# Folding the gate weights in full columns, with the spatial weights in one transfer

## The chip, the cores and the metric

The kernel runs on one core of a Trainium2 chip. The metric is the device time of one execution in microseconds (us), as the median of several runs; lower is better. The engines are TensorE (PE in the profile, its weight loads PEld), VectorE (DVE), ScalarE (ACT), GpSimd (POOL) and SyncE (SP). All arithmetic is float32.

## The reference

Three stages run one behind the other. The first is a recurrence over 768 time steps for 4 batches of 8 heads of width 40, the second a gated layer with a spatial mix, the third a routed layer with eight experts. Cut to what matters:

```python
def _attn_ref(r, k, v, w, a, b):                 # y: [4, 8, 768, 40]
    for t in range(S):
        y[:, :, t] = einsum('bhd,bhde->bhe', rt, state)
        Sa = einsum('bhde,bhe->bhd', state, at)
        state = state * wt - outer(Sa, bt) + outer(vt, kt)

def _moe_ref(x, w_in, w_spatial, b_spatial, w_out):
    h = maximum(x @ w_in, 0.0); u, v = halves of h            # 512 each
    v_n = (v - mean(v)) / sqrt(var(v) + 1e-6)
    v_s = einsum('ts,bsd->btd', w_spatial, v_n) + b_spatial[None, :, None]
    return (u * v_s) @ w_out                                  # [4, 768, 320]

def _moe2_ref(x, w_gate, w_local, w1, w2):
    logits = x @ w_gate; local_gate = sigmoid(x @ w_local)    # 8 and 1 columns
    e = argmax(logits) where fresh, otherwise the expert of the token before
    out = softmax(logits)[e] * (maximum(x @ w1[e], 0) @ w2[e])
```

## The kernel before

**The recurrence** (lines 948 to 1458) is cut into 24 chunks of 32 time steps. TensorE runs a loop of one step for each chunk (line 1175): small products with names like `unknowns`, `level`, `growth`, `scores_r`, `outputs`. In the profile a step takes 13.2 us. The other engines run the same chunks written out. SP loads each chunk's inputs (kb, a, vt, own, w, r and, last in a step, rg), each in a buffer of its own that is freed in the step. ScalarE copies banks of PSUM to SBUF (`drain`, line 1237), among them the state turned for the outputs, which also waits until rg has landed (line 1263). At one fixed place of each chunk it issues one part of the weights of the next stage (lines 1268 to 1272): `load` at line 124 has the spatial weights in six parts, `w_in` in four; `load_out` at line 139 the ten parts of the output and gate weights. VectorE masks the scores (line 1419) and scales the outputs (line 1455, it counts `y_d`).

**The end of the recurrence** is written out for TensorE in lines 1192 to 1215. Here the last chunk's products are mixed with the first products of the gated stage. `values` (line 230) multiplies two tiles of 128 tokens with the second half of `w_in` as a pair (`pair`, line 216): the full rows of the first tile, then whatever `between` holds, the full rows of the second tile, then the 64 remaining rows of both at line 227, side by side. Each tile of x waits for its own semaphore `x_tile`. The banks G and E of the first pair must have been read by ScalarE (`relu_v`, line 324) before the second pair writes them. The last tile of x is known only after the last outputs: `y_d`, then SP's `store` (line 935), then `load_tile` (line 938), and behind it on SP the bias and the first experts' weights. `gates` (line 247) multiplies the first half of `w_in`, with x streaming.

**The fold** (lines 163 to 190) computes w_out times the gate weights, a matrix of 512 rows by 9 columns (eight logits and one local gate), so that the output products of line 317 give the logits with the rows. w_out's transpose is in `woutT`, the nine columns in `wgl`, in three chunks of the 320 features (128, 128 and 64 rows). Twelve products load `wgl` as the stationary side and stream 128 columns of `woutT`, in four strips of 32 partitions of bank A. ScalarE copies the strips to SBUF (line 180), TensorE turns them (line 184), and ScalarE copies the result behind w_out (line 188). GpSimd adds the last weights for the mix behind this copy (line 269), since they take the place of `woutT`. The mix (`mix`, line 291) is the fourteen products of line 305.

The order in every engine's queue is the order in which the program is written. No scheduler moves anything.

Of the kernel before, what the change touches and what calls it, by code (L numbers as in the profile page):

```python
# [12 lines left out]
ACT = mybir.ActivationFunctionType  # L13
AX = mybir.AxisListType

P = 128
BATCH, HEADS, SEQ, HD = 4, 8, 768, 40
DM = HEADS * HD
# [5 lines left out]
EXPERTS = 8  # L24
# [51 lines left out]
class Gated:  # L76
# [4 lines left out]
    def __init__(self, nc, ctx, room, side, banks, x_rows, w_in, w_spatial, b_spatial, w_out, w_gate, w_local):  # L81
# [28 lines left out]
        self.transfers = TILES + 1 + NK  # L110
        self.strips, self.strips_clear = side.xTt[:, 0, 0, :], sem("strips_clear")
# [12 lines left out]
    def load(self, eng, part):  # L124
        w_in, w_spatial, b_spatial, w_out, w_gate, w_local = self.sources
        pairs = [(self.wspT[:, t, :], w_spatial[t * P:(t + 1) * P, :]) for t in range(TILES)]
# [36 lines left out]
    def fold(self, pe, woutT, wgl, bank, done):  # L163

        pe.wait_ge(self.out_loaded, 16 * self.OUT_PARTS)
        for k, (lo, rows) in enumerate(KCH):
            for d in range(ND):
                mm = pe.matmul(bank[self.strip(d), 0:P], wgl[0:rows, k, :], woutT[0:rows, k, d * P:(d + 1) * P],
                               start=(k == 0), stop=(k == NK - 1), skip_group_check=True)
        mm.then_inc(done, 1)  # L170

    def strip(self, d):

        return slice(d * 32, d * 32 + EXPERTS + 1)

    def copy_strips(self, act, bank, folded, done):
        act.wait_ge(folded, 1)
        act.wait_ge(self.strips_clear, 1)
        for d in range(ND):
            act.activation(self.strips[self.strip(d), :], bank[self.strip(d), 0:P], ACT.Copy).then_inc(done, 1)  # L180

    def turn_fold(self, pe, bank, ident, copied, done):
        pe.wait_ge(copied, ND)
        pe.transpose(bank[:, P:2 * P], self.strips, ident[:, :]).then_inc(done, 1)

    def copy_fold(self, act, bank, turned, done):
        act.wait_ge(turned, 1)
        act.activation(self.wout[:, :, DM:ROW],
                       bank[:, P:2 * P].rearrange("p (d n) -> p d n", n=32)[:, :, 0:EXPERTS + 1],
                       ACT.Copy).then_inc(done, 1)  # L190
# [39 lines left out]
    def values(self, pe, b, i, between=None):  # L230

        if b == 0:
            pe.wait_ge(self.x_tile[i], 16 * (NK + 1))
        if b >= 1 and i == 0:
            pe.wait_ge(self.x_full, 16 * (NK + 1) * b)

        def second():
            if between:
                between()
            if b == 0:  # L240
                pe.wait_ge(self.x_tile[i + 1], 16 * (NK + 1))

        self.pair(pe, self.v_at(b, i), D_HALF,
                  lambda g, k, rows: self.xT[rows, k, (i + g) * P:(i + g + 1) * P],
                  lambda g, k, rows: self.win[rows, k, D_HALF:], second)
# [1571 lines left out]
```

## Time and profile before

| | us |
|---|---|
| median of 3 runs | 933.83 |
| lowest and highest | 932.93, 934.34 |
| the profiled execution | 933.83 |
| its span, first to last instruction | 932.1 |
| TensorE busy in the span | 915.0 |
| recurrence, to the first values product | 347.5 |
| from there to the first gates product | 14.4 |
| from there to the first product of the mix | 19.1 |
| the rest: mix, batches 1 to 3, experts | 551.2 |

The span is what one execution took between its first and last instruction; the time of a run holds 1.7 us more. In the rows of the timeline the first number is the start in us from the span's start, the second how long the group lasted, then engine, line, operation and operands, and in brackets how long the engine was idle before it and what ended that. A float32 product shows as two passes, so x24 are twelve products.

### The profile page before, as it was taken

To read this page: it belongs to the slowest core of one execution; us is meant where nothing else is said; L and a number is where in the kernel's file an instruction comes from. 1 tells how busy PE (TensorE), PEld (TensorE's weight loads), DVE (VectorE), ACT (ScalarE), POOL (GpSimd) and SP (SyncE) were. 2 spreads that over 40 slices of the span, in tenths; PEclk is the share of its full clock that TensorE was granted. 3 is DMA by queue.
4 is the path that set the end of the run, shared out by engine and by line. 5 is a ranking of instruction groups with operands and counts; after the bars stand their busy time and mean duration, and the time that the engine had idled before them with its cause. 6 is when DMAs were issued, how large, how long until landed. Compare 5 with 4: busy or idle time off the path is not lost.

```text
span 932.1 us, 54066 instructions
## 1 busy us (share of the span) xinstructions
PE 915.0 (98%) x24654; PEld 710.4 (76%) x24655; DVE 477.5 (51%) x1026; ACT 251.5 (27%) x531; POOL 256.1 (27%) x232
## 2 busy tenths in 40 slices
PE   7999999999999999999999999999999999999997
PEld 6899999999999984545545545568888888888885
DVE  5478777877787643745455455463352222222230
ACT  0244444444444432102112112112212121212120
POOL 6454555455545551000020020020350111111011
PEclk8899999999999999999999999999999999999999
DMA  4235554554454322950110110329221110101000
GB/s 118 67 128 165 164 159 152 168 153 127 122 153 133 98 73 56 322 165 1 52 42 1 51 43 0 112 90 322 71 94 37 33 39 28 30 23 35 29 30 4
DMA packets 61477, 86.01 MB, mean 92 GB/s; under 512 B 22786, under 2 KB 41038, under 8 KB 61424
## 3 DMA queue, kind: packets, MB, share of 16 engines
q1 hardware_dynamic: 37232, 63.30, 22.2%
q10 hardware_dynamic: 21168, 13.32, 5.3%
q0 software_dynamic: 3024, 8.72, 2.6%
q8 instruction: 28, 0.46, 0.2%
q14 instruction: 25, 0.20, 0.1%
HBM read 72.47 MB, written 14.45 MB: 93 GB/s over the span
## 4 chain that ended last, share of the span: by engine, by line
PE 98%; issue 1%; ACT 0%; DVE 0%; POOL 0%; DVEq 0%; POOLq 0%; ACTq 0%
PE ps_D L1610 14%; PE ps_D L305 8%; PE ps_G L1592 6%; PE ps_E L1592 6%; PE ps_B L317 6%; PE ps_E L1096 5%; PE ps_A L305 4%; PE ps_B L223 3%; PE ps_G L1599 3%; PE ps_E L1094 3%; PE ps_D L1131 3%; PE ps_D L1068 3%; PE ps_G L223 3%; PE ps_D L1170 3%; PE ps_E L223 3%; PE ps_A L1073 2%
## 5 line engine op out<-in xcount | busy, mean ns | idle before, releaser
L1610 PE MATMUL ps_D<-room,hT 128*128 x496 | 138.8, 433 | 0.0
L1610 PEld LDWEIGHTS ps_D<-room,hT 128*128 128x128 f32 x496 | 91.9, 190 | 34.7
L1553 POOL DMA_INDIRECT out<-y,token x31 | 34.8, 1123 | 254.9 <-DVE y L1718 184.0
L661 POOL DMA_INDIRECT sorted_rows<-rows,slot x24 | 23.9, 995 | 237.7 <-DVE slot L653 231.6
L1718 DVE TENSOR_SCALAR y<-ps_D,x_in 128x320 f32<-128x320 f32 x31 | 17.0, 549 | 125.5 <-PE ps_D L1610 125.5
L1654 ACT ACTIVATE hT<-ps_G 128x512 f32<-128x512 f32 x31 | 18.5, 598 | 216.1 <-PE ps_E L1599 216.1
L1701 DVE COPY w_own<-room 128x1024 f32 x62 | 44.3, 720 | 63.0 <-PE ps_G L1592 34.4
L1350 DVE STREAM_TRANSPOSE room<-room 128x256 f32<-128x256 f32 x96 | 42.3, 441 | 48.1 <-ACT room L1237 48.1
L1592 PEld LDWEIGHTS ps_G<-xTt,w_own 128*128 128x128 f32 x496 | 60.0, 192 | 5.3 <-issue 1.0
L1592 PE MATMUL ps_G<-xTt,w_own 128*128 128x128 f32 x496 | 60.6, 275 | 0.6 <-ACT hT L1654 0.6
L1592 PE MATMUL ps_E<-xTt,w_own 128*128 128x128 f32 x496 | 60.5, 275 | 0.0
L1592 PEld LDWEIGHTS ps_E<-xTt,w_own 128*128 128x128 f32 x496 | 57.9, 192 | 0.0
L1019 POOL TENSOR_TENSOR room<-room 128x640 f32<-128x640 f32 x23 | 46.4, 2019 | 30.4 <-DVE room L1398 30.4
L317 PE MATMUL ps_B<-room 128*128 128x329 f32 x192 | 54.6, 441 | 0.0
L1237 ACT ACTIVATE room<-ps_E 128x256 f32<-128x256 f32 (+1 forms) x96 | 35.0, 365 | 66.9 <-PE ps_E L1096 36.6
L995 POOL TENSOR_TENSOR room<-room 128x1024 f32<-128x1024 f32 x24 | 52.2, 2176 | 1.9
L1030 POOL TENSOR_TENSOR room<-room 128x256 f32<-128x256 f32 x24 | 15.7, 656 | 125.7 <-DVE room L1442 125.7
L317 PEld LDWEIGHTS ps_B<-room 128*128 128x128 f32 x192 | 36.0, 190 | 18.4 <-issue 2.3
L1237 ACT ACTIVATE room<-room 128x512 f32<-128x512 f32 (+2 forms) x72 | 40.2, 558 | 34.5 <-PE ps_B L1148 31.2
L1096 PE MATMUL ps_E<-room 32*32 32x48 f32 (+1 forms) x3200 | 48.0, 205 | 1.5 <-issue 1.5
L1096 PEld LDWEIGHTS ps_E<-room 32*32 32x32 f32 x3200 | 40.6, 104 | 7.0 <-issue 6.0
L1237 ACT ACTIVATE room<-ps_D 128x1024 f32<-128x1024 f32 x24 | 24.6, 1026 | 48.6 <-PE ps_D L1068 48.6
(260 smaller groups left out, 1769.8 us busy)
## 6 DMA issues: line engine op xcount, KB each, us to landing
room<-in_moe_w SPq DMA_DIRECT2D x8, 1280.0 KB, 14.0
room<-in_moe_w SPq DMA_DIRECT2D x8, 1024.0 KB, 11.3
room<-in_vt SPq DMA_DIRECT2D x24, 320.0 KB, 3.8
room<-in_kb SPq DMA_DIRECT2D x46, 160.0 KB
x_in<-sorted_rows ACTq DMA_DIRECT2D x27, 161.0 KB, 2.2
room<-in_vo SPq DMA_DIRECT2D x24, 160.0 KB, 4.0
room<-in_rg SPq DMA_DIRECT2D x48, 80.0 KB
room<-in_r SPq DMA_DIRECT2D x48, 80.0 KB
```

Source lines behind the costliest of these rows:

```text
L223: pe.matmul(self.bank_of(n + g)[:, 0:width], left(g, k, slice(0, P)), right(g, k, slice(0, P)), start=(k == 0), stop=False, skip_group_che ...
L305: mm = pe.matmul(self.vs_bank[n % 3][:, 0:TH], left[:, s, c * P:(c + 1) * P], right[:, s, :], start=(s == 0), stop=(s == ST - 1))
L317: mm = pe.matmul(self.o_bank[n % 2][:, 0:ROW], self.g[:, d, i * P:(i + 1) * P], self.wout[:, d, :], start=(d == 0), stop=(d == ND - 1))
L995: pool.tensor_tensor(kb_end.rearrange("p m n k t -> p (m n) k t"), raw_kb[:, :, :, :], later[:, :, None, :].broadcast_to([P, GROUPS, 2, CH ...
L1019: pool.tensor_tensor(faded.rearrange("p m n e -> p (m n) e")[:, :, 0:HD], stateT.rearrange("p m n e -> p (m n) e"), whole[:, x % 4, :, Non ...
L1096: mm = pe.matmul(E[q, :, i, kept], pw[q, i, :], powers[q, l - 2:ROUNDS - 1:ROUNDS - l, i, kept], start=True, stop=True)
L1237: act.activation(out, in_, ACT.Copy).then_inc(done, 1)
L1350: dve.transpose(pw.rearrange("p i t -> p (i t)"), (powers[:, l - 1] if l else qi[:, 0]).rearrange("p i t -> p (i t)")).then_inc(flip_d[l], 1)
L1553: pool.indirect_dma_start(out=self.out[:, :], out_offset=bass.IndirectOffsetOnAxis(ap=side.token[:, u:u + 1], axis=0), in_=side.y[:, u % 2 ...
L1592: mm = pe.matmul(self.ps_h[half][:, f, :], side.w1_own[:, k, col:col + P], x[:, k, :], start=(f == 0 and k == 0), stop=False, skip_group_c ...
L1610: mm = pe.matmul(self.ps_y[:, u % 2], side.hT[:, u % 2, f, :], self.weights.w2[:, bass.ds(e, 1), f, :], start=(f == 0), stop=(f == self.NF ...
L1701: dve.tensor_copy(side.w1_own[:, :, cols], w1.w1[:, bass.ds(e, 1), :, cols].rearrange("p o k f -> p (o k) f")).then_inc(self.w1_in, 1)
```

## The change

Three things are edited. The six transfers of the spatial weights become one of 2304 KB, issued in the place of the first, so that the later parts of the weights are each issued five steps earlier. The fold loads `woutT` as the stationary side, 128 columns at a time, and streams the nine columns of `wgl`; its result stands on all 128 partitions as it is wanted, and the strips, their copies, the turning and the fill of the strips go. On TensorE the scores of the last chunk come in front of the second pair of values, the last outputs between its halves, and each pair of values waits for both of its tiles at its start.

```diff
-        self.transfers = TILES + 1 + NK
-        self.strips, self.strips_clear = side.xTt[:, 0, 0, :], sem("strips_clear")
+        self.transfers = 2 + NK
...
-        pairs = [(self.wspT[:, t, :], w_spatial[t * P:(t + 1) * P, :]) for t in range(TILES)]
+        pairs = [(self.wspT[:, :, :], w_spatial.rearrange("(t p) s -> p t s", p=P))]
...
-        for k, (lo, rows) in enumerate(KCH):
-            for d in range(ND):
-                mm = pe.matmul(bank[self.strip(d), 0:P], wgl[0:rows, k, :], woutT[0:rows, k, d * P:(d + 1) * P],
-                               start=(k == 0), stop=(k == NK - 1), skip_group_check=True)
+        for d in range(ND):
+            for k, (lo, rows) in enumerate(KCH):
+                mm = pe.matmul(bank[:, d, 0:EXPERTS + 1], woutT[0:rows, k, d * P:(d + 1) * P], wgl[0:rows, k, :],
+                               start=(k == 0), stop=(k == NK - 1))
...
-    def copy_strips(self, act, bank, folded, done):
+    def copy_fold(self, act, bank, folded, done):
         act.wait_ge(folded, 1)
...
-    def turn_fold(self, pe, bank, ident, copied, done):
...
+        act.activation(self.wout[:, :, DM:ROW], bank[:, :, 0:EXPERTS + 1], ACT.Copy).then_inc(done, 1)
...
-        if b == 0:
-            pe.wait_ge(self.x_tile[i], 16 * (NK + 1))
+        for t in (i, i + 1):
+            if b == 0:
+                pe.wait_ge(self.x_tile[t], 16 * (NK + 1))
...
-                pool.memset(gated.strips, 0.0).then_inc(gated.strips_clear, 1)
...
-                gated.fold(pe, woutT, wgl, A[:, 1], folded)
-                gated.values(pe, 0, 2, lambda: scores_r(now))
-                pe.wait_ge(kt_d, CHUNKS)
-                pe.wait_ge(rvu_d, now)
-                outputs(now)
-                pe.wait_ge(routing.consts, routing.CONSTANTS)
-                gated.turn_fold(pe, A[:, 1], side.ident, strips_d, fold_turned)
+                gated.fold(pe, woutT, wgl, A[:, 1].rearrange("p (d n) -> p d n", n=P), folded)
+                scores_r(now)
+
+                def final_outputs():
+                    pe.wait_ge(kt_d, CHUNKS)
+                    pe.wait_ge(rvu_d, now)
+                    outputs(now)
+
+                gated.values(pe, 0, 2, final_outputs)
...
-                gated.relu_v(act, 0, 1)
-                gated.copy_strips(act, A[:, 1], folded, strips_d)
-                for i in range(2, 4):
+                for i in range(1, 4):
                     gated.relu_v(act, 0, i)
-                gated.copy_fold(act, A[:, 1], fold_turned, fold_d)
+                gated.copy_fold(act, A[:, 1].rearrange("p (d n) -> p d n", n=P), folded, fold_d)
```

TensorE's queue at the end of the recurrence, from the fold to the first gates product. Before (L168 is the fold, L223 and L227 are values or gates, L1131 the scores, L1148 the outputs, L184 the turning):

```order
L168 MATMUL ps_A<-w_own 9x128 x11
L223 MATMUL ps_G<-room 128x512 [waits h_out,x_tile2]
L223 MATMUL ps_G<-room 128x512
L1131 MATMUL ps_D<-room 64x32 [waits vu_d_drained]
L1131 MATMUL ps_D<-room 64x32 x31
L223 MATMUL ps_E<-room 128x512 [waits x_tile3]
L223 MATMUL ps_E<-room 128x512
L227 MATMUL ps_G<-room 128x512
L227 MATMUL ps_E<-room 128x512
L1148 MATMUL ps_B<-room 40x32 [waits rvu_drained,kt_drained]
L1148 MATMUL ps_B<-room 40x32 x31
L184 MATMUL ps_A<-ident,xTt 128x128 [waits strips_d,rt_consts]
```

The same place after the change; the new file's lines are some 17 to 24 lower (L167 the fold, L1107 the scores, L206 and L210 values, L1124 the outputs):

```order
L167 MATMUL ps_A<-w_own 128x9 x11
L1107 MATMUL ps_D<-room 64x32 [waits vu_d_drained]
L1107 MATMUL ps_D<-room 64x32 x31
L206 MATMUL ps_G<-room 128x512 [waits h_out,x_tile3,x_tile2]
L206 MATMUL ps_G<-room 128x512
L1124 MATMUL ps_B<-room 40x32 [waits rvu_drained,kt_drained]
L1124 MATMUL ps_B<-room 40x32 x31
L206 MATMUL ps_E<-room 128x512 x2
L210 MATMUL ps_G<-room 128x512
L210 MATMUL ps_E<-room 128x512
L206 MATMUL ps_D<-room 128x384 x4
```

The scores and the outputs have moved ahead by half a pair of values each, the turning is gone, and both tile waits of a pair stand at its start.

ScalarE's queue in the first step that has a part of the weights. Before:

```order
L1237 ACTIVATE room<-ps_B 104x640 [waits fT_filled,ld_rg]
L1237 ACTIVATE room<-room 128x512 [waits a_end_d,rh_filled]
L1237 ACTIVATE room<-ps_E 128x256 [waits round1_filled]
L130 DMA room<-in_moe_w_spatial 128x768
L1237 ACTIVATE room<-ps_D 128x1024 [waits vT_filled,ld_r]
```

After:

```order
L1215 ACTIVATE room<-ps_B 104x640 [waits fT_filled,ld_rg]
L1215 ACTIVATE room<-room 128x512 [waits a_end_d,rh_filled]
L1215 ACTIVATE room<-ps_E 128x256 [waits round1_filled]
L129 DMA room<-in_moe_w_spatial 128x6x768
L1215 ACTIVATE room<-ps_D 128x1024 [waits vT_filled,ld_r]
```

The order around the transfer is unchanged; it is six times as large, and the five like it in the next steps give their places to the parts that followed.

## Rows read from the trace of the kernel before

**Rows 1.** The page's fourth part: the chain that ended last, by engine.
```profile
PE 98%; issue 1%; ACT 0%; DVE 0%; POOL 0%; DVEq 0%; POOLq 0%; ACTq 0%
```

**Rows 2.** TensorE's waits: us in total, times, longest.
```profile
PE ps_G L223 <- ACT room L324: 0.9, 1, 0.9
```

**Rows 3.** Timeline of TensorE, from the fold to the third pair of values.
```profile
353.18 0.96 PE L168 MATMUL ps_A<-w_own 128*9 128x128 f32 x24
355.00 1.95 PE L223 MATMUL ps_G<-room 128*128 128x512 f32 x4 [0.87 <-ACT room L324]
356.89 1.14 PE L1131 MATMUL ps_D<-room 64*64 64x32 f32 x64
357.95 1.98 PE L223 MATMUL ps_E<-room 128*128 128x512 f32 x4
...
360.93 0.81 PE L1148 MATMUL ps_B<-room 64*40 64x32 f32 x64
361.67 0.33 PE L184 MATMUL ps_A<-ident,xTt 128*128 128x128 f32 x1
361.84 2.75 PE L223 MATMUL ps_D<-room 128*128 128x384 f32 x8
...
368.99 1.98 PE L223 MATMUL ps_G<-room 128*128 128x512 f32 x4
370.81 1.88 PE L223 MATMUL ps_E<-room 128*128 128x512 f32 x4
```

**Rows 4.** Timeline of ScalarE, VectorE and SP there; last, the page's DMA issues.
```profile
353.35 1.02 ACT L1237 ACTIVATE room<-ps_D 128x1024 f32<-128x1024 f32 x1 [0.45 <-PE ps_D L1068]
354.27 0.59 ACT L324 ACTIVATE room<-ps_E 128x512 f32<-128x512 f32 x1
358.09 0.69 DVE L1419 TENSOR_TENSOR room<-ps_D,room 128x512 f32<-128x512 f32 x1 [10.72 <-PE ps_D L1131]
367.69 0.60 SPq L155 DMA_DIRECT2D room<-x_rows  x1
...
room<-x_rows SPq DMA_DIRECT2D x12, 32.0 KB, 2.0
```

**Rows 5.** Line 168's weight loads (ns min/median/max), and busy time in its stretch.
```profile
L168 PEld LDWEIGHTS ps_A<-w_own x24: 82/88/91, 353.2 to 353.8; 128*9 128x9 f32 x16, 64*9 64x9 f32 x8
...
353.18:353.98 0.80, 0.80 (x25) 0.45 (x24) 0.00 (x0) 0.63 (x1) 0.00 (x0) 1.00 0.00 0
```

**Rows 6.** Timeline of the weight loads at line 631, and their durations in ns.
```profile
465.95 0.30 PEld L631 LDWEIGHTS ps_A<-onehot,ones 128*128 128x128 f32 x2
466.17 0.30 PEld L305 LDWEIGHTS ps_D<-room 128*128 128x128 f32 x2
...
L631 PEld LDWEIGHTS ps_A<-onehot,ones x8: 192/192/192, 466.0 to 666.1; 128*128 128x128 f32 x8
```

**Rows 7.** Two steps (clock, DMA share, GB/s at the end); line 130's issues.
```profile
42.15:55.33 13.18, 13.13 (x858) 12.06 (x857) 10.25 (x21) 4.74 (x10) 7.16 (x6) 1.00 0.36 113
55.33:68.51 13.18, 13.13 (x858) 12.06 (x857) 10.25 (x21) 5.78 (x11) 7.02 (x6) 1.00 0.44 143
...
L130 ACTq DMA_DIRECT2D room<-in_moe_w_spatial x6: 353/364/396, 57.2 to 123.1; - x6
```

**Rows 8.** Timeline of two steps of the recurrence: ScalarE's drains, and TensorE behind one.
```profile
59.70 1.03 ACT L1237 ACTIVATE room<-ps_D 128x1024 f32<-128x1024 f32 x1 [2.09 <-PE ps_D L1068]
...
68.84 0.70 ACT L1237 ACTIVATE room<-ps_B 104x640 f32<-104x640 f32 x1 [0.69 <-DMA room<-in_rg]
...
305.92 0.79 PE L1108 MATMUL ps_A<-room 32*32 32x40 f32 x64
306.95 0.70 ACT L1237 ACTIVATE room<-ps_B 104x640 f32<-104x640 f32 x1 [1.38 <-DMA room<-in_rg]
307.88 0.73 PEld L1142 LDWEIGHTS ps_B<-room 64*40 64x40 f32 x64 [0.28 <-issue]
```

**Rows 9.** Issues of expert weights on SP, line 433: ns min/median/max.
```profile
L433 SPq DMA_DIRECT2D room<-in_moe_w x32: 390/596/8008, 369.0 to 639.5; - x32
```

More of the change, by code:

```diff
@@ L165, in fold @@
         pe.wait_ge(self.out_loaded, 16 * self.OUT_PARTS)
-        for k, (lo, rows) in enumerate(KCH):
-            for d in range(ND):
-                mm = pe.matmul(bank[self.strip(d), 0:P], wgl[0:rows, k, :], woutT[0:rows, k, d * P:(d + 1) * P],
-                               start=(k == 0), stop=(k == NK - 1), skip_group_check=True)
+        for d in range(ND):
+            for k, (lo, rows) in enumerate(KCH):
+                mm = pe.matmul(bank[:, d, 0:EXPERTS + 1], woutT[0:rows, k, d * P:(d + 1) * P], wgl[0:rows, k, :],
+                               start=(k == 0), stop=(k == NK - 1))
         mm.then_inc(done, 1)
-    def strip(self, d):
-        return slice(d * 32, d * 32 + EXPERTS + 1)
-    def copy_strips(self, act, bank, folded, done):
+    def copy_fold(self, act, bank, folded, done):
         act.wait_ge(folded, 1)
-        act.wait_ge(self.strips_clear, 1)
-        for d in range(ND):
-            act.activation(self.strips[self.strip(d), :], bank[self.strip(d), 0:P], ACT.Copy).then_inc(done, 1)
-    def turn_fold(self, pe, bank, ident, copied, done):
[L183 to L190, printed above, removed]
+        act.activation(self.wout[:, :, DM:ROW], bank[:, :, 0:EXPERTS + 1], ACT.Copy).then_inc(done, 1)
     V_FIRST = {0: (0, 1, 4), 1: (0, 1, 2)}
@@ L230, in values @@
     def values(self, pe, b, i, between=None):
-        if b == 0:
-            pe.wait_ge(self.x_tile[i], 16 * (NK + 1))
+        for t in (i, i + 1):
+            if b == 0:
+                pe.wait_ge(self.x_tile[t], 16 * (NK + 1))
         if b >= 1 and i == 0:
             pe.wait_ge(self.x_full, 16 * (NK + 1) * b)
[L237 to L241, printed above, removed]
         self.pair(pe, self.v_at(b, i), D_HALF,
                   lambda g, k, rows: self.xT[rows, k, (i + g) * P:(i + g + 1) * P],
-                  lambda g, k, rows: self.win[rows, k, D_HALF:], second)
+                  lambda g, k, rows: self.win[rows, k, D_HALF:], between)
     def gates(self, pe, b, j):
@@ L850, in all_stages @@
         passed = sem("waits_passed")
-        folded, fold_d, strips_d, fold_turned = (sem(x) for x in ("folded", "fold_d", "strips_d", "fold_turned"))
+        folded, fold_d = sem("folded"), sem("fold_d")
         steps = range(-3, CHUNKS)
```

## The prediction, made before the changed kernel had run

> **What bounds the kernel now.** I read the page's fourth part first, the chain of work that ended last: it is 98% TensorE [rows 1]. So a change is worth what it does to TensorE's own stream: how many microseconds of matmuls it puts in or takes out, and which waits it opens or closes there. In the list of TensorE's waits the longest outside the start-up is 0.9 us in front of a values product at line 223 [rows 2], and the change touches that place. Next I read TensorE's timeline from the end of the recurrence (the loop over 24 chunks) to the middle of batch 0 of the gated stage [rows 3], and beside it what the other engines do there [rows 4]. The reader is to see that TensorE is gapless except for that 0.87 us at 355.00, which is spent until ScalarE has read the first two value tiles out of the banks G and E (354.27 + 0.59 = 354.86).
>
> The profiled execution took 933.83 us, of which 932.1 us are the span; it is also the median of the three runs (932.93 to 934.34). So I add differences of the span to 933.83.
>
> **The fold (terms 1 and 2).** Before, twelve products load nine columns as the stationary side and stream 128, and their results go to four strips of 32 partitions each; four strips run side by side. 24 passes (a float32 product shows as two) start at 353.18, and the window from there to 353.98 holds 24 weight loads in only 0.45 us of busy time [rows 5]: I take 0.80 us from the first pass to the point at which the next instruction could start. Afterwards each product loads 128 columns, streams nine, and writes all 128 partitions, so no two can run side by side. The nearest row is the counting product at line 631: it loads 128x128 float32 and streams 48 columns. Its first load starts at 465.95, after two of them line 305 loads at 466.17 [rows 6]: 0.11 us a pass. 24 passes give 24 x 0.11 = 2.64 us, an addition of 1.84 us. Nothing in the trace streams only nine columns behind a full load. The bounds are the strips' own loads, 88 ns each [rows 5] (24 x 0.088 = 2.11 us), and a load that nothing hides, 192 ns at line 631 [rows 6] (24 x 0.192 = 4.61 us). I take 2.64, because the row at 0.11 differs from the new product only in streaming 48 columns and not nine. A cost as low as before (0.80) would need the products side by side, which the output on all partitions excludes.
>
> The Trainium skill, TensorE: Matmul & The Clock Gate, in its part on packing small matmuls, says that products with few output rows gain from being placed in different column strips, 2.38 times with three of them; this speaks against the change. The 0.45 us of loads in rows 5 agree with it. By that factor, and up to three for four strips, the new fold would take an estimated 1.9 to 2.4 us, and the sum below would come to -0.1 to +0.4 us.
>
> What goes away: the 0.87 us of idle time, since a longer fold and the scores now stand in front of the values product; the turning of the strips, 0.17 us between lines 184 and 223 [rows 3]; four strip copies on ScalarE, a fill on GpSimd, and the wait for the identity, which all lie beside TensorE's work and count nothing.
>
> **The new order.** Take the steps from start to start in rows 3. The first half of the values product is 356.89 - 355.00 = 1.89, the scores 357.95 - 356.89 = 1.06, the second half with the two remainders 360.93 - 357.95 = 2.98, the outputs 361.67 - 360.93 = 0.74. From the fold's start to the first gates product it is now 361.84 - 353.18 = 8.66 us. Afterwards it is 2.64 (fold) + 1.06 + 1.89 + 0.74 + 2.98 = 9.31 us, if nothing waits. **So +0.65 us.** Do the waits fit?
> - The scores wait for ScalarE's drain of the turned vu, done at 353.35 + 1.02 = 354.37 [rows 4]. The fold ends at 355.82, so this is covered by 1.4 us. If the fold were short, this wait would be the next one: the scores could not start before about 354.5.
> - The values product waits for the drain that ends at 354.86, and starts at 356.88.
> - The outputs wait for VectorE's mask over the scores. It starts 358.09 - 356.89 = 1.20 us after them and takes 0.69 [rows 4]: ready at 355.82 + 1.89 = 357.71. They start at 355.82 + 1.06 + 1.89 = 358.77, covered by 1.1 us of the first half that now stands between.
> - The outputs come 2.16 us earlier than at 360.93. So do VectorE's drain, the store, and the load of the last x tile on SP, whose last issue is now at 367.69 and whose kind lands in 2.0 us [rows 4]: about 369.7 before, 367.5 after. The pair of values at 368.99 now waits for both of its tiles in front of the first half instead of between the halves. It starts at 362.49 + (368.99 - 361.84) = 369.64, so the wait is 2.1 us away. Before, the tile was wanted at 370.81 [rows 3], with 1.1 us to spare. The earlier load buys nothing, since nobody waits for it; nor do the expert weights behind it on SP.
> - The fold's copy now stands behind the second pair's drains on ScalarE. GpSimd's last weight sum, which waits for it, comes some 1.3 us later. It is wanted only by the fifth product of the mix, behind the values pair of 368.99 and two more pairs of gates; cover of over 10 us.
>
> **The weight load (term 3).** Six transfers of 384 KB, one in each of six steps of the recurrence, become one of 2304 KB in the first, and all later weight parts come five steps earlier. TensorE does not wait for any of them, so being earlier earns nothing. The question is what the large one disturbs. In the step of 55.33 to 68.51, the first with a piece, the 16 DMA engines were busy 0.44 of 13.18 us, in the step before without one 0.36 [rows 7]: about 1.05 us of all sixteen for each piece. Five more add 5.3 us, so the step holds 0.44 x 13.18 + 5.3 = 11.1 us of 13.2. It is issued at 57.2 [rows 7] and fits only just before the step's end. The transfer that is short of slack is the raw rg block, the last one of the step. ScalarE's drain at 68.84 waits for it [rows 8], and TensorE needs that drain at line 1142. The trace shows the price of a late one. The drain at 306.95 is 1.03 us behind its step's start (305.92), and TensorE's next weights wait 0.28 us; the drain at 68.84 is 0.33 us behind its own (68.51) [rows 8]. So about 0.45 us of delay is free, and beyond that each costs its length. From about 58.2, a microsecond behind the issue, 11.1 us of work would end at about 69.3, where the block was in at 68.8. If the two queues share evenly, a delay of up to 0.5 us is what I expect; unshared it is zero. I take **+0.1 us**, with ends 0 and +0.6. The other blocks of the step (kb, a, vt, own, w, r) are wanted several microseconds later. ScalarE's issue of the large transfer may take longer than the 0.36 us of a piece [rows 7]; its next work is at 59.70 [rows 8], 2.5 us away.
>
> Sum: 0.65 + 0.1 = 0.75 us, 933.83 + 0.75 = **934.6 us**.
>
> **The rivals.**
> 1. *The fold comes cheap.* If the loads pace at 88 ns or below, TensorE waits for the scores' operand at 354.5, and the stretch is 1.3 + 6.67 = 8.0 us: 0.67 less at best, so 933.2 us; at 88 ns 0.1 more, 933.9. For it: nine columns stream faster than 48. Against it: at line 631 the weight load already sets the pace, and it is the same. Chance 0.08.
> 2. *The loads are not hidden.* 4.61 us of fold, +2.62 us: 936.5, slower by 0.3%. For it: one load by itself takes 0.19 us [rows 6]. Against it: the same rows show 0.11 from load to load. Chance 0.03.
> 3. *ScalarE is held by the large transfer.* This one ends on the slow side. SP's issues of expert weights took 0.60 us in the middle and 8.0 us at most [rows 9], when the queue was full. At 57.2 an issue longer than 2.5 us delays the drain that the scores need in that step; 8.0 us would cost 5.5, 940.2 us. Or the rg block lands more than 1.7 us late, which costs over 1.2 us: 935.7 or more. For it: six times the descriptors at once. Against it: at 57.2 ScalarE's queue is empty, and the median row of larger transfers is 0.60. The Trainium skill, DMA: Bandwidth & Descriptors, on queues and rings, says that an engine drains a whole packet, typically 9 to 17 descriptors, from one ring before it turns to the next. If the rg block had to wait one such turn, an estimated 1.2 to 2.2 us (a piece's 1.05 us of sixteen engines over its 128 rows is 0.13 us a descriptor), the time would be 0.7 to 1.8 us longer; no row here tells packets apart. Chance 0.07.
> 4. *The joined wait bites.* If the last tile does not come earlier, it lands at 369.7 against a start at 369.64, and up to 0.7 us at the worst landing is lost: 935.3 at most. Decides from a landing later than 369.6. Chance 0.04.
> 5. *Something that I don't see gives more than 1.9 us.* The only idle time in reach is 0.87 us. Chance 0.03.
>
> **How the numbers follow.** The forecast has a chance of 0.75. About 0.2% (1.9 us) is what a measurement here can tell from no change. Same: forecast, rivals 1 and 4, 0.87. Slower: rivals 2 and 3, 0.10. Faster: rival 5, 0.03. The range goes from rival 1 less the runs' spread below their median (933.2 - 0.4 = 932.8) to the unhidden loads, 936.4.
>
> **What would show it.** In the profile after: 24 passes of the fold about 0.11 us apart, some 2.6 us long; no gap in front of the scores nor the values product behind; the first gates product 9.3 us behind the fold's start; the values pair at 369.6 without a wait; steps of 13.18 us in the recurrence, with the third (68.5) at most 0.5 longer. Wrong if the fold takes under 2 or over 3 us, if a step of the recurrence grows by over 0.5 us, or if TensorE waits for the x tile.

## The result: 941.2 us, 0.9% slower, and the profile after

The changed kernel takes 941.17 us (median of 4 runs, 939.70 to 943.19) against 933.72 before: a ratio of 1.0087 with an interval of 1.0072 to 1.0103. That is 7.4 us slower; forecast were 0.75 us, and the time lies outside the range. Ten executions of it are on record, from 939.70 to 943.29, with a median of 941.7. Its profiled execution took 940.78 us, with a span of 939.0; the span of before was 932.1, so the 6.9 us between them can be looked for in the two traces.

The chain of the page's fourth part is still TensorE's, with one new entry: the DMA.

```profile
PE 97%; issue 1%; DMA 1%; ACT 0%; DVE 0%; POOL 0%; SPq 0%; DVEq 0%; POOLq 0%; ACTq 0%
```

**The step behind the large transfer.** Four steps of the recurrence, the second of them with the large transfer (columns: start and end, length, busy time of PE, PEld, DVE, ACT and POOL, granted clock, DMA share, GB/s); then TensorE's waits (total, times, longest):

```profile
41.41:54.57 13.16, 13.11 (x857) 12.06 (x856) 10.23 (x21) 4.74 (x10) 7.14 (x6) 1.00 0.37 113
54.57:67.75 13.18, 13.13 (x857) 12.05 (x856) 10.26 (x21) 5.81 (x11) 7.01 (x6) 1.00 0.75 246
67.75:83.68 15.93, 13.18 (x857) 12.08 (x856) 10.25 (x21) 5.70 (x11) 7.02 (x6) 1.00 0.59 185
83.68:96.86 13.18, 13.13 (x857) 12.06 (x856) 10.25 (x21) 5.80 (x11) 7.02 (x6) 1.00 0.50 151
```
```profile
PE ps_B L1118 <- ACT room L1215: 3.3, 2, 2.7
```

The step of 54.57 has the same length as in [rows 7], and its DMA share is 0.75 where before it was 0.44. The next one is 2.75 us longer than before, and TensorE's busy time in it is not: it waits. Whom for stands in the timelines of SP, ScalarE and TensorE, with the page's line on the large transfer (last number: us from issue to landing) behind them:

```profile
65.63 0.66 SPq L854 DMA_DIRECT2D room<-in_rg  x2
```
```profile
56.50 0.45 ACTq L129 DMA_DIRECT2D room<-in_moe_w_spatial  x1
...
58.96 1.03 ACT L1215 ACTIVATE room<-ps_D 128x1024 f32<-128x1024 f32 x1 [2.08 <-PE ps_D L1044]
...
71.30 0.70 ACT L1215 ACTIVATE room<-ps_B 104x640 f32<-104x640 f32 x1 [3.88 <-DMA room<-in_rg]
```
```profile
72.31 0.81 PE L1118 MATMUL ps_B<-room 64*40 64x32 f32 x64 [2.69 <-ACT room L1215]
```
```profile
room<-in_moe_w_spatial ACTq DMA_DIRECT2D x1, 2304.0 KB, 13.4
```

SP issues the rg block at 65.63 as ever, 2.12 us before the step's end. ScalarE's drain that wants it starts at 71.30, 5.7 us behind the issue; in the trace of before the issue is at 66.38 and the drain at 68.84 [rows 8], 2.5 us. The large transfer is in the engines from 56.5 to 69.9, and from 58.5 to 66.6 all sixteen are full (share 0.99 to 1.07 in windows of 1 to 2 us). An earlier block on SP's queue was late as well: `in_vo` (160 KB), issued at 60.42, landed after 7.7 us, in the same step before after 2.7 us. So the block was 3.2 us later than before, and TensorE paid 2.7 of it. ScalarE itself was not held: its issue took 0.45 us.

**From the fold to the first gates product.** The timeline of TensorE, to be laid beside [rows 3]:

```profile
355.42 4.11 PE L167 MATMUL ps_A<-w_own 128*128 128x9 f32 x24
359.46 1.93 PE L1107 MATMUL ps_D<-room 64*64 64x32 f32 x64
361.32 3.58 PE L206 MATMUL ps_G<-room 128*128 128x512 f32 x4
364.83 0.81 PE L1124 MATMUL ps_B<-room 64*40 64x32 f32 x64
365.57 1.98 PE L206 MATMUL ps_E<-room 128*128 128x512 f32 x4
...
368.55 0.59 PE L206 MATMUL ps_D<-room 128*128 128x384 f32 x1
```

There is no gap, as forecast, but everything up to 364.83 is longer than it should be: the fold 4.04 us, the scores 1.86 (before 1.06), the first half of the values 3.51 (before 1.89). The reason stands in the column of the granted clock of the same stretches:

```profile
355.42:357.00 1.58, 1.58 (x14) 1.52 (x12) 0.00 (x0) 1.32 (x2) 0.00 (x0) 1.00 0.00 0
357.00:359.46 2.46, 2.46 (x14) 2.34 (x14) 0.00 (x0) 0.19 (x1) 0.00 (x0) 0.65 0.00 0
359.46:361.32 1.86, 1.86 (x66) 1.79 (x65) 0.00 (x0) 0.00 (x0) 0.00 (x0) 0.50 0.00 0
361.32:364.83 3.51, 3.51 (x9) 1.17 (x5) 0.69 (x1) 0.00 (x0) 0.00 (x0) 0.54 0.00 0
364.83:368.55 3.72, 3.72 (x74) 1.68 (x73) 2.56 (x11) 0.00 (x0) 0.00 (x0) 1.00 0.27 58
```

From 357.7 to 364.6, 2.3 us into the fold and then for 6.8 us, TensorE was granted 0.50, the lower of its two levels (1.2 instead of 2.4 GHz). In all the recurrence behind the start-up it had been at 1.00, and the profile shows it busy all the time before the fall.

**The ledger of the two spans**, in us after minus before: start-up to the second step -0.74 (41.41 against 42.15); from there to the fold +2.98, of which 2.75 are the long step; fold to first gates +4.47 (13.13 against 8.66); gates to mix +0.10; the rest +0.14. Sum 6.95.

### The profile page after: what moved, and what is told of

It is laid out like the page before. It is cut to its first block, busy times and chain, and to the rows that moved or that the text cites. A ratio compares the mean times of both kernels' runs of the same rounds, so it can differ in the third digit from the quotient of the medians.

```text
span 939.0 us, 54053 instructions
## 1 busy us (share of the span) xinstructions
PE 919.0 (98%) x24653; PEld 713.8 (76%) x24654; DVE 475.2 (51%) x1026; ACT 250.4 (27%) x527; POOL 255.7 (27%) x231
## 4 chain that ended last, share of the span: by engine, by line
PE 97%; issue 1%; DMA 1%; ACT 0%; DVE 0%; POOL 0%; SPq 0%; DVEq 0%; POOLq 0%; ACTq 0%
PE ps_D L1586 14%; PE ps_D L282 8%; PE ps_G L1568 6%; PE ps_E L1568 6%; PE ps_B L294 6%; PE ps_E L1072 5%; PE ps_A L282 4%; PE ps_B L206 3%; PE ps_G L1575 3%; PE ps_D L1107 3%; PE ps_D L1044 3%; PE ps_E L1070 3%; PE ps_G L206 3%; PE ps_E L206 2%; PE ps_D L1146 2%; PE ps_A L1049 2%
## 5 line engine op out<-in xcount | busy, mean ns | idle before, releaser
L1694 DVE TENSOR_SCALAR y<-ps_D,x_in 128x320 f32<-128x320 f32 x31 | 17.1, 550 | 125.5 <-PE ps_D L1586 125.5
```

## Experiments

Each was timed against the kernel before on the same chip, where that one had medians of 934.15 to 935.51 us; "ratio" is to its time there. The step from the fold's start to the first gates product is called the stretch (before 8.66 us, after 13.13). None of these kernels leaves anything of the computation out.

### One part alone: the transfer, the fold, the order

**The changed kernel with six transfers again.**

```diff
-        self.transfers = 2 + NK
+        self.transfers = TILES + 1 + NK
...
-        pairs = [(self.wspT[:, :, :], w_spatial.rearrange("(t p) s -> p t s", p=P))]
+        pairs = [(self.wspT[:, t, :], w_spatial[t * P:(t + 1) * P, :]) for t in range(TILES)]
```

> The changed kernel with the spatial weights in six transfers again, one a step. Theory (the large transfer takes the rg block's bandwidth and holds one step of the recurrence up by 2.75 us): no step longer than 13.5 us, time 941.2 - 2.75 = 938.4 us, 0.5% over the kernel before. Rival (the long step has another cause, such as the changed places of the later parts): a step of about 16 us remains, 941 us. The stretch from the fold to the first gates product should stay at 13.1 us in both.

Measured: 937.08 us (935.32 to 939.44, 10 runs) against 934.15, ratio 1.0028 (1.0017 to 1.0039). No step of the recurrence behind the start-up is over 13.3 us, so the long one is the transfer's. The profiled execution, with 939.44 the slowest of the ten, has a stretch of 13.13 again:

```profile
354.22 4.05 PE L167 MATMUL ps_A<-w_own 128*128 128x9 f32 x24
358.20 1.93 PE L1107 MATMUL ps_D<-room 64*64 64x32 f32 x64
360.06 3.64 PE L206 MATMUL ps_G<-room 128*128 128x512 f32 x4
```

**The kernel before with the large transfer only** (the two lines above, in the other direction).

> The kernel before with the spatial weights in one transfer and nothing else. Theory: one step of the recurrence of 15.9 us instead of 13.2 and all else as before, 933.7 + 2.75 = 936.5 us. Rival (the transfer alone is harmless, the two edits together make the step long): 933.8 us.

Measured: 937.62 us (937.07 to 939.65, 5 runs), ratio 1.0040 (1.0025 to 1.0054). The stretch is 8.66 as before. The step behind the transfer takes 17.73 us. Two windows show it whole and its dearest part:

```profile
68.72:86.45 17.73, 14.72 (x859) 13.42 (x858) 10.24 (x21) 5.79 (x11) 7.00 (x6) 0.90 0.56 169
...
74.60:78.10 3.50, 3.50 (x98) 3.09 (x89) 2.19 (x3) 0.95 (x1) 2.34 (x2) 0.51 0.75 212
```
```profile
PE ps_B L1142 <- ACT room L1237: 3.4, 2, 3.0
```

The same wait takes 3.0 us here, and behind it the granted clock is at 0.50 for 3.4 us, which adds some 1.6. So the stall has a price of its own (2.7 to 3.3 us in the six profiles with the whole transfer in one step) and in some executions that of the clock behind it.

**The old fold in strips with the new order and the large transfer.**

> The changed kernel with the fold in four strips again, copied and turned as before; one transfer and the new order stay. Theory (TensorE's clock falls to its lower level behind the slow nine-column fold): no fall at the end of the recurrence, the stretch from the fold to the first gates product takes 1.3 + 6.7 + 0.2 = 8.2 us instead of 13.1, time 941.2 - 4.9 = 936.3 us. Rival (the fall of the clock comes from the new order, or from where the stretch happens to lie): the clock falls all the same, 940 us or more.

Measured: 936.89 us (936.54 to 937.75, 6 runs), ratio 1.0032 (1.0019 to 1.0044). The long step is there (17.60, with 0.50 from 73.3 to 76.7), the stretch is 8.20, and no fall of the clock stands at its end.

**The new order and the joined waits only** (strips, six transfers).

```diff
...
-                gated.values(pe, 0, 2, lambda: scores_r(now))
-                pe.wait_ge(kt_d, CHUNKS)
-                pe.wait_ge(rvu_d, now)
-                outputs(now)
+                scores_r(now)
...
+                gated.values(pe, 0, 2, final_outputs)
```

> The kernel before with the new order and both tile waits at a pair's start; six transfers and the fold in strips. Theory: the stretch takes 8.2 us instead of 8.66, all else as before: 934.15 - 0.46 = 933.7 us, which a measurement can hardly tell from no change. Rival: a wait of the new order shows on the chip (for the last tile, for the scores' operand), 934.5 us or more.

Measured: 933.72 us (932.15 to 934.53, 11 runs) against 934.51, ratio 0.9995 (0.9986 to 1.0004): no difference that could be told.

```profile
353.86 0.96 PE L168 MATMUL ps_A<-w_own 128*9 128x128 f32 x24
355.19 1.14 PE L1127 MATMUL ps_D<-room 64*64 64x32 f32 x64 [0.38 <-ACT room L1237]
356.26 1.98 PE L223 MATMUL ps_G<-room 128*128 128x512 f32 x4
358.17 0.81 PE L1144 MATMUL ps_B<-room 64*40 64x32 f32 x64
```

The order closes the wait of 0.87 us in front of the values and opens one of 0.38 in front of the scores, as the working of the waits said for a short fold. The stretch is 8.20, which is 0.46 less.

**The new fold in the old order, with the joined waits, six transfers** (one run).

> The kernel before with the fold in full columns and with both tile waits at a pair's start, in the old order and with six transfers. Theory: the fold's passes go at 0.11 us where the rows stay 128, with 0.1 us more at each change between 128 and 64 rows, 3.4 us at the upper clock level; the values product follows at once. The clock may fall during the fold as in two profiles with the new order (4 us of fold then), since the fold is what those have in common and the order is not: stretch to the first gates product 8.66 - 0.87 - 0.17 - 0.8 + 3.4 = 10.2 us without a fall, about 13 us with one. Rival on the clock (the small products of the scores right behind the fold are needed for the fall): no fall. Rival on the waits: the joined wait holds the third pair of values back, by up to 0.7 us.

Measured: 936.15 us. This execution shows the new fold without any fall of the clock:

```profile
352.95 3.40 PE L167 MATMUL ps_A<-w_own 128*128 128x9 f32 x24
356.28 1.98 PE L206 MATMUL ps_G<-room 128*128 128x512 f32 x4
358.20 1.14 PE L1107 MATMUL ps_D<-room 64*64 64x32 f32 x64
...
371.18 1.10 PE L206 MATMUL ps_G<-room 128*128 128x512 f32 x2 [0.88 <-issue]
```

From the fold's start to the next product it takes 3.33 us, 0.69 more than forecast. In the start times of its 24 passes 0.11 us lie between passes of the same row count, and 0.32 instead of 0.22 over two steps wherever the loads change between 128 and 64 rows, which they do seven times. The last row is another finding: in the old order the pair of values now starts 0.88 us late. The row names nothing that it waited for; that it is the second tile is inferred: the last issue of its load is at 368.98, such loads land in 2.0 us, and in the next kernel, with the old waits, the gap is not there. So the joined wait costs something by itself, and the new order hides it.

**The new fold alone, in the old order with the old waits.**

> The kernel before with the fold in full columns and nothing else: old order, old waits, six transfers. Theory (as one profile of the old order showed): no fall of the clock, the stretch from the fold to the first gates product 10.0 us instead of 8.66, and no wait for the last tile: 934.2 + 1.4 = 935.6 us. Rival (the fall comes with this fold in any order, only by chance not in that one profile): runs spread up to 938 us and a fall in the profile.

Measured: 936.16 us (934.60 to 938.42, 10 runs), ratio 1.0018 (1.0007 to 1.0030). The runs stand in two groups, seven from 934.6 to 936.3 and three from 938.1 to 938.4, of which the profiled one is one. Its stretch, and the same one of the kernel above:

```profile
352.93:366.18 13.25, 13.25 (x166) 7.82 (x165) 0.69 (x1) 2.11 (x4) 0.00 (x0) 0.74 0.00 0
```
```profile
352.95:362.98 10.03, 10.03 (x166) 6.54 (x165) 0.69 (x1) 2.11 (x4) 0.00 (x0) 1.00 0.00 0
```

TensorE's work in the two is the same 166 matmuls in the same order, and 3.22 us lie between them: the clock alone, 0.74 against 1.00. The fall comes in the old order as in the new one, and the two groups of run times say that it comes in some executions and not in others.

### What about the transfer does the harm

**Six pieces of 384 KB, issued back to back in one step** (one run).

```diff
-        pairs = [(self.wspT[:, :, :], w_spatial.rearrange("(t p) s -> p t s", p=P))]
+        pairs = [tuple((self.wspT[:, t, :], w_spatial[t * P:(t + 1) * P, :]) for t in range(TILES))]
...
```

> The changed kernel with the spatial weights in six transfers of 384 KB, all issued one behind the other at the place of the large one. Theory (what counts is how much lies on ScalarE's queue in one step, since SP's transfers get only their share of the engines while it lasts): the rg block of that step comes some 3 us late again, the step takes 15.9 us or more, as with one transfer. Rival (the size of a single transfer is what counts): every step 13.2 to 13.3 us.

Measured: 942.24 us. The steps are 13.65 and 17.70 (a wait of 3.0 us, and behind it 3.4 us at a clock of 0.50), so small pieces do the same: what matters is how many bytes are in flight beside the rg block. A second effect can be seen in the first of the two steps, in ScalarE's and TensorE's timelines:

```profile
56.15 3.04 ACTq L129 DMA_DIRECT2D room<-in_moe_w_spatial  x6
59.30 1.03 ACT L1215 ACTIVATE room<-ps_D 128x1024 f32<-128x1024 f32 x1 [2.77 <-PE ps_D L1044]
```
```profile
60.47 1.14 PE L1107 MATMUL ps_D<-room 64*64 64x32 f32 x64 [0.42 <-ACT room L1215]
```

Six issues hold ScalarE for 3.04 us, and the scores wait 0.42 us for the drain behind them.

**Two parts of 1152 KB in two steps.**

> The changed kernel with the spatial weights in two transfers of 1152 KB in two steps. Theory (a backlog on SP's queue that has until the rg block to clear): each lands some 7 us behind its issue, SP catches up before the rg block, no step over 13.5 us; the time is that of the kernel with six parts, 937 us. Rival (any transfer larger than a piece delays the rg block beyond its slack): two steps of over 14 us, 939 us or more.

Measured: 938.07 us (938.03 to 938.66, 4 runs), ratio 1.0042 (1.0027 to 1.0058). The step behind the first part takes 14.14 us, 0.96 too long, but not for the rg block, which is in (ScalarE's drain waits 0.87 us for it, where 0.69 is usual). ScalarE's and TensorE's timelines:

```profile
70.34 0.42 ACTq L130 DMA_DIRECT2D room<-in_moe_w_spatial  x1
70.80 3.08 ACTq L848 DMA_DIRECT2D x_rows<-room  x2
73.98 1.02 ACT L1216 ACTIVATE room<-ps_D 128x1024 f32<-128x1024 f32 x1 [3.26 <-issue]
```
```profile
75.15 1.14 PE L1108 MATMUL ps_D<-room 64*64 64x32 f32 x64 [0.91 <-ACT room L1216]
```

Behind the second part, ScalarE's two stores of y (line 848) take 3.08 us to issue. In the kernel after they took 0.93 us together, at 72.15, when the large transfer was in and one of 512 KB had been issued 0.4 us before. The drain of the scores' operand stands behind them, and TensorE waits 0.91 us for it. The rest of the loss is in the stretch: 11.62 us, with the clock at 0.50 for 3.4 of them. Neither side had it right: the rg block is on time, as the theory said, but the parts cost a microsecond by another way.

**The large transfer issued at the end of its step**, where most blocks of the step are in.

```diff
-                    if 1 <= c <= gated.transfers:
+                    if 2 <= c <= gated.transfers:
...
                         drain(cols(kb_tok), cols(kb_next[:, x % 2]), kn_d, x + 1, kt_d)
+                    if c == 1:
+                        gated.load(act, 0)
```

> The changed kernel with the one large transfer issued at the end of the same step, just behind the rg block's issue, instead of in its first third. Theory (the rg block is late because SP's queue has a backlog of half a step when its turn comes): 13.4 us of flight now end at about the next rg block's issue, so the next step is at most 0.5 us longer and the time some 3 to 4 us lower than the changed kernel's, 937.5 us. Rival (a transfer of this size delays whatever SP sends, wherever it starts): a step of 15 us or more, 941 us.

Measured: 940.40 us (939.99 to 941.84, 4 runs), ratio 1.0064 (1.0046 to 1.0082); a step of 16.08. The idea that a late issue is harmless fell. SP's and ScalarE's timelines say why:

```profile
67.15 0.67 SPq L854 DMA_DIRECT2D room<-in_rg  x2
```
```profile
67.16 0.46 ACTq L129 DMA_DIRECT2D room<-in_moe_w_spatial  x1
73.01 0.70 ACT L1215 ACTIVATE room<-ps_B 104x640 f32<-104x640 f32 x1 [4.08 <-DMA room<-in_rg]
```

The two issues fell on the same moment, and the rg block (160 KB in two transfers) took 5.9 us instead of 2.5. Until then SP's queue had run as in the kernel before, so there was no backlog of earlier blocks in front of it. The two queues between 68.5 and 73.0, while the rg block was out (packets, MB, share of the engines; q10 is ScalarE's, known by its packets of 3 KB, the rows of the large transfer, and q1 is SP's):

```profile
q10 hardware_dynamic: 457, 1.40, 92.5%
q1 hardware_dynamic: 65, 0.09, 5.6%
```

It is the sharing of the engines while the large transfer flies that makes the block late, wherever in the step the flight begins. In the kernel after a backlog came on top (the late `in_vo`), but the block is as late without one.

### What about the fold does the harm

**The nine columns padded with zeros to 128 streamed ones**, with the large transfer and, later, with six.

```diff
-                mm = pe.matmul(bank[:, d, 0:EXPERTS + 1], woutT[0:rows, k, d * P:(d + 1) * P], wgl[0:rows, k, :],
+                mm = pe.matmul(bank[:, d, :], woutT[0:rows, k, d * P:(d + 1) * P], wgl[0:rows, k, :],
...
```

> The changed kernel with the nine streamed columns of the fold filled up with zeros to 128, so that the loads are the same and each pass streams more; the result in the nine columns is the same. Theory (few streamed columns let the clock fall): the clock stays at 1.0, a pass takes 0.12 us, the fold 2.9 us, the stretch to the first gates product 9.6 us, time 941.2 - 3.5 = 937.7 us. Rival (full weight loads, one by one, are what makes the fold slow or lets the clock fall): fold of 4 us, 941 us or more.

Measured: 939.77 us (939.25 to 941.21, 4 runs), ratio 1.0057 (1.0041 to 1.0074). I expected a fold of 2.9 us; it took 4.13, but at full clock, so the stretch was 10.82, 2.3 us less than with nine columns. (Its step behind the transfer takes 18.13, with a wait of 3.3 us and 3.4 us at 0.50.) What makes this fold long stands in the start times of its passes: 0.11 us between those of one row count, and 0.42 instead of 0.22 over two steps at each of the seven changes of the row count, 0.20 more at each:

```profile
358.28 4.20 PE L167 MATMUL ps_A<-w_own 128*128 128x128 f32 x24
362.41 1.14 PE L1108 MATMUL ps_D<-room 64*64 64x32 f32 x64
```
```profile
358.28:369.10 10.82, 10.82 (x166) 6.54 (x164) 3.25 (x12) 1.51 (x2) 0.00 (x0) 1.00 0.09 20
```

> The fold with its nine columns padded by zeros to 128 streamed columns (the result is the same), and the spatial weights in six transfers, so that nothing disturbs the recurrence. Stretch from the fold's start to the first gates product 10.8 us as in the padded kernel with one transfer, 2.2 more than before: about 936.3 us by the shared median of 934.1. Theory A, the clock falls because a product behind a full load streams only nine columns: no fall in any execution, so the run times lie close together (within 1.5 us) and each run's mean granted clock is about the same as before's (0.991 to 0.997). Theory B, the clock falls because of the full-column loads or the pause between the stages, however many columns are streamed: some of the runs are 2 to 4 us above the others, at a mean clock of 0.983 to 0.988, and a profile may show 0.50 for 3.4 or 6.8 us behind the fold.

Measured: 936.79 us (935.30 to 938.55, 10 runs) against 935.51, ratio 1.0016 (1.0006 to 1.0027). The stretch is 10.82 again at a clock of 1.00, as forecast. The ten runs lie within 3.3 us, not within 1.5, but the kernel before itself spread over 3.8 us on this chip, and they form no second group. The mean clock of the ten is 0.989 twice and 0.991 to 0.995 eight times, and before's was 0.989 to 0.996. The two runs at 0.989 are among the three slowest, as a fall would have it. But the mean clock can't tell: in the start-up alone the 15 profiles show 0.50 for between 6.8 and 17.1 us in all, a spread of 10 us, where 3.4 or 6.8 are looked for. Two padded profiles without a fall lean towards the theory that only the nine-column form is followed by it, and don't settle it.

**The chunks of the sum in the outer loop**, so that the row count of the loads changes once and not seven times (six transfers).

```diff
-        for d in range(ND):
-            for k, (lo, rows) in enumerate(KCH):
+        for k, (lo, rows) in enumerate(KCH):
+            for d in range(ND):
...
-                               start=(k == 0), stop=(k == NK - 1))
+                               start=(k == 0 and d == 0), stop=(k == NK - 1), skip_group_check=True)
```

> The changed kernel with six transfers, and the fold's twelve products with the row chunks in the outer loop, so that products of 64 rows stand together (one change of the row count instead of seven). Theory: the extra 0.1 us at each change goes, the fold takes 24 x 0.111 + 0.3 = 2.9 us instead of 3.3 at the upper clock level, and the stretch 9.6 us without a fall of the clock, some 12.6 with one. Rival (64-row loads are slow in themselves): fold of 3.3 us still. Whether the clock falls with a fold this short is open; if it does, the few columns matter and not the fold's length.

Measured: 935.26 us (934.66 to 939.54, 10 runs) against 934.55, ratio 1.0016 (1.0001 to 1.0031). The fold takes 2.77 us to the next product, its passes 0.112 us apart but for the one change, even in an execution whose clock falls behind it:

```profile
354.14 2.84 PE L167 MATMUL ps_A<-w_own 128*128 128x9 f32 x24
356.91 1.14 PE L1107 MATMUL ps_D<-room 64*64 64x32 f32 x64
357.97 3.23 PE L206 MATMUL ps_G<-room 128*128 128x512 f32 x4
```

Against 3.33 us that is 0.56 for six changes less, 0.09 each. The stretch is 11.06. Six of the ten runs are at 934.7 to 935.4, and the others at 936.3, 937.3, 939.1 and 939.5; the last three have the lowest mean clocks (0.991, 0.989, 0.983).

**The fold behind the third pair of values**, between dense products (six transfers).

> The changed kernel with six transfers and the same fold moved behind the third pair of values, so that products with 384 and 512 streamed columns stand on both sides of it, and the scores no longer follow it. Theory on the clock (the clock falls where the fold and the small products of the turning and the scores stand together): no fall, from the last fold-free start to the mix 8.2 - 0.17 - 0.6 + 19.1 + 3.3 us, time 934.2 - 0.5 + 3.1 = 936.5 us in every run. Rival (the nine-column fold alone brings the fall): a stretch at the lower level behind it, with 512-column products at half speed, 938 us or more.

Measured: 937.49 us (936.75 to 938.95, 6 runs), ratio 1.0041 (1.0027 to 1.0054), though the profiled execution has no fall. The forecast of this run, 936.5, is missed by 1 us; one profile can't say whether its slower runs hold a fall. Two rows of TensorE's timeline show what else it costs:

```profile
354.26 1.36 PE L1107 MATMUL ps_D<-room 64*64 64x32 f32 x64 [1.27 <-ACT room L1215]
```
```profile
373.12 3.50 PE L167 MATMUL ps_A<-w_own 128*128 128x9 f32 x24
```

The fold was what hid ScalarE's drain in front of the scores. Taken away from there, it leaves a wait of 1.27 us behind, and costs its 3.4 us in the other place as well.

## Why the prediction was wrong, point by point

- **What bounds the kernel**: right. Every loss found is one of TensorE's stream: a wait, passes, or a slower clock.
- **The fold's pitch**: 0.11 us from the row at line 631 was right for passes of one shape. The step that failed is "24 x 0.11": the twelve products alternate between 128 and 64 rows, and each of seven changes costs another 0.09 us or so (the kernel with one change: 2.77 us). 3.33 us instead of 2.64, so **+0.7 us**. The one row with 0.11 showed a run of 128-row loads only; the row counts stood in the code. On the Trainium skill's packing rule (TensorE: Matmul & The Clock Gate, Part 3) the text took the row against the rule, and rightly for the size, since the rule's 1.9 to 2.4 us were too low; its direction, that the strips are the faster form, is what these runs show (0.80 against 3.33 us).
- **The order**: right. With the fold's real length the sum gives 9.31 + 0.69 = 10.00 us for the stretch, and the rows of the order-only kernel with a fold of 3.33 us put in give 10.03 (8.20 - 0.17 of turning - 1.33 + 3.33). The waits that were said to be covered are covered, the pair of values starts at 375.79, 20.37 us behind the fold, without a wait, and the joined wait alone (0.88 us in the old order) is what rival 4 described, hidden here by the earlier outputs as forecast.
- **The clock**: a term that the forecast put at nothing without a reason. The working added durations at the clock of the rows that it took them from. Between 10.03 and 13.13 us, both profiled, lie **3.1 us**: 0.7 in the fold, 0.8 in the scores, 1.6 in the values. Of eight profiles with nine streamed columns at the end of the recurrence seven show the fall (6.8 us in five, 3.4 in two) and one does not; of six profiles with strips or 128 columns there none does. The ten runs of the fold alone, three of them some 2.5 us above the rest, say that it depends on the execution. In the run times it is also rarer than in the profiles: three of these ten, three of ten with the chunks outside. So 3.1 us is its price where it comes; the six-transfer kernel's median is only 1.6 us above what the stretch of 10.03 would give (937.08 - 934.15, less the 1.37 from 8.66 to 10.03). TensorE shows as busy all through the fold in either case, so the share of busy time could not have told it. The Trainium skill (the same page, Part 1) has the clock follow how busy the array has been, and half the clock as the state of an idle one; here no idle time stands in front of the fall, but passes that stream nine columns behind a load of 128. That the form of the fold is what the clock answers to is the likeliest reading, and is not shown: it rests on eight profiles against six, two of them padded, of something that comes and goes. Which property of it (the few streamed columns, or something that the padding changed with them) stays open.
- **The weight load**: the step that failed is "a delay of up to 0.5 us is what I expect". It asked whether the step's work fits in the engines' time (11.1 of 13.2 us, done at 69.3, 0.8 us behind the step's end) and took equal sharing. The share in the step was 0.75, and the transfer flew to 69.9, 2.1 us behind the end of its step. But the rg block doesn't need the engines' total; it needs its own turn within 2.5 us of its issue, and where both queues had work they did not share equally (0.09 MB against 1.40 in the kernel with the late issue). The block took 5.7 us. The price put on a late block was right: 3.2 us late less the 0.45 us that are free is 2.75, the length by which the step grew. This is the second arm of rival 3 (over 1.7 us late, 935.7 or more), which was given 0.07; its first arm, ScalarE held while it issues, shows in the kernels with six pieces in one step (3.04 us) and with two parts (3.08 us). The price by itself is **+3.5 us** (ratio 1.0040), of which 2.7 to 3.3 are the wait and the rest the clock behind it in those executions where it fell. Taken from the kernel after (941.17 - 933.72 = 7.4) less the six-transfer kernel (937.08 - 934.15 = 2.9), it is 4.5. On the Trainium skill's rule that a DMA engine drains a whole packet of one ring before it turns to the next (DMA: Bandwidth & Descriptors, Queues, rings and completion order), the text estimated 1.2 to 2.2 us for one turn; the block was 3.2 us later than before, in the direction of that rule and beyond its one turn.
- **The sum**: 0.65 of the stretch as forecast, 0.7 for the changes of row count, 3.1 for the clock and 2.75 for the late block, where 0.1 had been put, are 7.2 us; with the start-up at -0.74 and small ones at +0.47 this is the ledger's 6.95 (within rounding). Three of the prediction's sums are off by 0.1 us and change nothing: rival 3's 940.2 should be 940.1, the unhidden loads give 936.5 in rival 2 and 936.4 in the range, and the estimate of -0.1 to +0.4 us leaves out the transfer's 0.1.
- **The range**: its upper end was worked out from loads that nothing hides (936.4). Even with the six-transfer fold the median of 937.08 is above it. A fault of method: the bounds were put around the terms that I had, not around those for which the trace of before had no row.

What the change gives on its good side is small: the order alone is 0.46 us better in the profile, within the uncertainty of the runs. No kernel here is faster than the one before by more than that uncertainty.

## What to carry to other kernels

When a transfer is made larger or moved, ask which small transfer with short slack is issued while it flies, and compare its slack (here 2.5 us from issue to use) with the large one's whole flight (13.4 us), not the engines' total work with the length of the step. When small matmuls are put in another form, count the changes of row count between loads as well as the passes. And a stall, or a fold of the form used here, can be paid for twice, the second time by the clock of the work behind it: compare the granted clock of the same stretch in several executions before a loss is put down to the code.

## What was not expected of the hardware

- Two hardware queues do not share evenly by bytes in this trace: with 2304 KB in flight on ScalarE's queue, 160 KB on SP's took 5.7 us instead of 2.5, and 5.9 us when the large transfer was issued only at the same moment as they. In 4.5 us of that ScalarE's queue moved 1.40 MB and SP's 0.09.
- A change between loads of 128 and of 64 rows costs about 0.09 us of TensorE's time with nine streamed columns (seven changes, 3.33 against 2.77 us with one). With 128 streamed columns a change costs about 0.20 us: the fold takes 4.13 us with seven of them, and its other passes are 0.11 us apart as well.
- The granted clock fell to 0.50 for 3.4 or 6.8 us inside or behind a fold of 24 passes with nine streamed columns, without idle time in front of it, in seven of eight profiles; and behind a stall of about 3 us in a loop that had otherwise kept it at 1.00 (a fall behind stalls of 2.8 to 3.3 us in four profiles, none behind 2.7 and 2.8 us in two, and none in the loop of the nine without such a stall).
- Two issues of stores on ScalarE took 3.08 us behind a transfer of 1152 KB on its queue, where they took 0.93 behind one of 512 KB.
